# Expert stage of an attention and mixture-of-experts kernel: tiles of 64 slots instead of 128

## What is computed

```python
logits = x @ w_gate                       # 1792 x 768 @ 768 x 8
e_idx = np.argmax(logits, axis=1)
...
for e in range(E):
    mask = e_idx == e
    h = np.maximum(x[mask] @ w1[e], 0.0)  # 768 -> 1024
    ye = h @ w2[e]                        # 1024 -> 768
    out[mask] = gate_w[mask, None] * eom[mask, e, None] * ye
```

## Time and profile before

| | us |
|---|---|
| median of 3 runs (lowest to highest) | 1076.08 (1074.73 to 1076.96) |
| profiled execution, its own time | 1077.28 |
| span of the profiled execution | 1075.2 |
| TensorE busy | 1055.4 |
| VectorE / ScalarE / GpSimd busy | 560.1 / 428.6 / 256.6 |
| expert stage, first matmul to last | 765.9 to 1067.7 |

### The profile page before, as it was taken

One profiled execution on the slowest core, in us unless ns is written; L12 is line 12 of the kernel. 1 busy time (PEld: TensorE's weight loads), 2 busy tenths in 40 slices (PEclk: granted clock), 3 DMA queues, 4 the chain that ended last, 5 costly groups with the idle time before them and its releaser, 6 DMA issues.

```text
span 1075.2 us, 20947 instructions
## 1 busy us (share of the span) xinstructions
PE 1055.4 (98%) x8120; PEld 621.7 (58%) x8121; DVE 560.1 (52%) x830; ACT 428.6 (40%) x611; POOL 256.6 (24%) x219
## 2 busy tenths in 40 slices
PE   7999999999999999999999999999999999899997
PEld 3444334444555555555555555556787887778785
DVE  7899999984433344433333321004455456266651
ACT  6788888886211111111111220001254444246531
POOL 5887878841000000000000100000121121122222
PEclk9999999999999999999999999999999999999999
DMA  6267867541411111111100432000366357357620
GB/s 159 59 140 139 174 146 166 118 95 36 149 44 51 54 51 54 49 54 58 59 30 1 162 104 81 36 29 30 137 221 247 118 209 246 106 199 286 215 95 19
DMA packets 117610, 118.89 MB, mean 111 GB/s; under 512 B 71600, under 2 KB 93486, under 8 KB 117536
## 3 DMA queue, kind: packets, MB, share of 16 engines
q1 hardware_dynamic: 113952, 106.37, 33.9%
q0 software_dynamic: 3168, 11.02, 2.9%
q10 hardware_dynamic: 416, 0.47, 0.2%
HBM read 99.49 MB, written 13.85 MB: 105 GB/s over the span
## 4 chain that ended last, share of the span: by engine, by line
PE 83%; POOL 8%; issue 7%; ACT 1%; DVE 0%; DMA 0%; POOLq 0%; ACTq 0%
PE ps L1695 30%; PE ps L1710 15%; PE ps L1766 14%; PE ps L1774 13%; PE ps L1591 5%; POOL arena L662 3%; PE ps L1565 2%; POOL arena L648 1%; PE ps L1754 1%; POOL arena L652 1%; POOL arena L669 1%; PE ps L1542 1%; PE ps L1582 1%; PE ps L1567 1%; DMA arena<-in_qk 0%
## 5 line engine op out<-in xcount | busy, mean ns | idle before, releaser
L1695 PE MATMUL ps<-arena 128*128 128x448 f16 x1728 | 328.8, 352 | 0.0
L1695 PEld LDWEIGHTS ps<-arena 128*128 128x128 f16 x1728 | 168.2, 98 | 156.1 <-issue 0.5
L1710 PE MATMUL ps<-arena 128*128 128x392 f16 (+1 forms) x996 | 165.3, 329 | 0.0
L1766 PE MATMUL ps<-arena 128*128 128x128 f16 x2592 | 149.1, 220 | 2.9 <-DVE arena L1267 2.9
L1766 PEld LDWEIGHTS ps<-arena 128*128 128x128 f16 x2592 | 147.5, 98 | 5.6 <-DVE arena L1267 3.3
L1774 PE MATMUL ps<-arena 128*128 128x384 f16 x864 | 146.3, 326 | 0.0
L1710 PEld LDWEIGHTS ps<-arena 128*128 (+1 forms) x996 | 97.3, 98 | 66.9
L1267 DVE SCALAR_TENSOR_TENSOR arena<-arena 128x768 f16<-128x768 f32 (+1 forms) x112 | 112.8, 1067 | 38.3 <-ACT arena L973 37.5
L940 ACT ACTIVATE arena<-ps 128x448 f32<-128x448 f32 x48 | 26.1, 543 | 257.8 <-PE ps L1695 257.8
L1591 PE MATMUL ps<-arena 128*128 128x448 f32 x288 | 126.6, 562 | 0.0
L1241 DVE SCALAR_TENSOR_TENSOR arena<-ps,arena 128x448 f32<-128x448 f32 x48 | 30.0, 625 | 171.5 <-PE ps L1695 92.7
(11 more groups left out here) (184 smaller groups left out, 962.7 us busy)
## 6 DMA issues: line engine op xcount, KB each, us to landing
arena<-in_moe_w SPq DMA_DIRECT2D x48, 512.0 KB, 3.8
arena<-in_moe_w SPq DMA_DIRECT2D x64, 384.0 KB, 3.9
arena<-in_qk SPq DMA_DIRECT2D x23, 448.0 KB, 4.5
y_parts<-arena SPq DMA_DIRECT2D x16, 384.0 KB, 2.3
arena<-sums_inv SPq DMA_DIRECT2D x48, 112.0 KB, 2.9
arena<-in_v SPq DMA_DIRECT2D x24, 192.0 KB, 2.9
arena<-in_moe_w_gate SPq DMA_DIRECT2D x12, 384.0 KB, 4.4
arena<-in_moe_w_val SPq DMA_DIRECT2D x12, 384.0 KB, 5.5
```

Source lines behind the costliest of these rows:

```text
L1695: last = nc.tensor.matmul(ps[:, 2 * (b % 2) + g, 0:S], up_w[s][:, g, c, wl], xt[:, b * KC + c, xl], start=(c == 0 and wl + xl == 0), stop= ...
L1710: last = nc.tensor.matmul(ps[:, 4 + 2 * s + h, 0:cols], gt[:, f, gl, bass.ds(t * 128, 128)], wo[:, f, wl, h, 0:cols], start=(f == 0 and gl ...
L1766: last = nc.tensor.matmul(ps[:, b, k * 128:(k + 1) * 128], w1_s[s][:, c, wl, f * 128:(f + 1) * 128], x_t[:, xl, c], start=(c == 0 and k == ...
```

## The change

A tile has 64 slots instead of 128, and an expert has at least three tiles. Of a tile's 128 gathered rows, 64 are the high parts and 64 the low parts of its tokens (`y_dram` is read as half rows of 1536 bytes, and `row_idx` holds twice the row's number plus 0 or 1). Six transposes turn them, and the first layer has 64 moving columns for each matmul. In the second layer the hidden values are 64 columns of weights; the matmul for the left half of the output columns goes to PSUM partitions 0 to 63 and that for the right half to 64 to 127 of the same bank, one after the other as a pair. So one eviction of 384 columns and one scatter of 128 half rows empties a tile, the last one too. The pieces of the next expert's weights are split in its predecessor's first three tiles: 5, 5 and 4 of them (0, 7 and 7 for expert 0), no longer in its own. Room is made for 49 tiles, so routing's tables grow from 22 to 49 entries for each token tile.

```diff
-CONST_COLS = 468
+CONST_COLS = 511
+SLOTS = 64
+SLOT_TILES = 49
...
-        x_rows = ym.take(128, 2 * DM, F16)
-        x_t = ym.take(128, 2 * DM, F16).rearrange("p (l c m) -> p l c m", l=2, c=KC)
+        x_rows = ym.take(128, DM, F16)
+        x_t = ym.take(128, DM, F16).rearrange("p (c l m) -> p c l m", l=2, c=KC)
...
-        hid = m2.take(128, F2, F32)
-        hid_t = m2.take(128, 2 * F2, F16).rearrange("p (b l c m) -> p b l c m", b=2, l=2, c=4)
+        hid = m2.take(128, F2 // 2, F32)
+        hid_t = m2.take(128, F2, F16).rearrange("p (b l c m) -> p b l c m", b=2, l=2, c=4)
...
-        out_rows = Region(xt_at, xt_at + 6144).take(128, DM, F32)
+        out_rows = Region(xt_at, xt_at + 6144).take(128, HALF_DM, F32)
...
-                many = eng.value_load(counts_i[0:1, bass.ds(e, 1)], min_val=1, max_val=TT)
+                many = eng.value_load(counts_i[0:1, bass.ds(e, 1)], min_val=3, max_val=2 * TT)
...
-                tile(e, s, before, True)
-                with eng.If(many > 1):
+                for i in range(3):
+                    tile(e, s, before + i, i)
+                with eng.If(many > 3):
                     if is_at(e, 0):
-                        with eng.Fori(0, many - 1) as i:
-                            tile(e, s, i, False)
+                        with eng.Fori(2, many - 1) as i:
+                            tile(e, s, i, None)
                     else:
-                        with eng.Fori(1, many) as i:
-                            tile(e, s, before + i, False)
+                        with eng.Fori(3, many) as i:
+                            tile(e, s, before + i, None)
...
+        def pieces_ahead(e, i):
+
+            if i is None or is_at(e, E - 1):
+                return ()
+            bounds = (0, 0, 7, PIECES) if is_at(e, 0) else (0, 5, 10, PIECES)
+            return tuple(range(bounds[i], bounds[i + 1]))
...
-                nc.gpsimd.indirect_dma_start(out=x_rows, out_offset=None, in_=y_dram,
+                nc.gpsimd.indirect_dma_start(out=x_rows, out_offset=None, in_=y_halves,
...
-                nc.gpsimd.indirect_dma_start(out=out, out_offset=bass.IndirectOffsetOnAxis(ap=scatter_idx, axis=0),
+                nc.gpsimd.indirect_dma_start(out=out_halves, out_offset=bass.IndirectOffsetOnAxis(ap=scatter_idx, axis=0),
...
-            for h in range(2):
-                cols = slice(h * HALF_DM, (h + 1) * HALF_DM)
-                pool.wait_ge(half_idx_ready, 2)
-                pool.wait_ge(last_out_ready, h + 1)
...
+            scatter(last)
...
             def hidden(g, b):
 
                 act.wait_ge(hid_sum, 2 * g + b + 1)
                 wait(act, hid_lo_ready, 2 * g)
-                nc.scalar.activation(hid[:, b * 512:(b + 1) * 512], ps[:, b, :], ACT.Relu, scale=1.0 / S_OP)\
+                nc.scalar.activation(hid[:, b * 256:(b + 1) * 256], ps[:, b, 0:256], ACT.Relu, scale=1.0 / S_OP)\
                     .then_inc(hid_ready, 1)
...
-                if first:
-                    split_high(e, s, range(KC + 5, PIECES) if is_at(g, 0) else range(KC, KC + 4))
+                if is_at(g, 0):
+                    split_high(e, s, range(KC + 5, PIECES))
                 hidden(g, 0)
-                if first and not is_at(g, 0):
-                    split_high(e, s, range(KC + 4, PIECES))
                 hidden(g, 1)
-                if first and not is_at(e, E - 1):
-                    split_high(e + 1, 1 - s, range(KC))
+                split_high(e + 1, 1 - s, pieces_ahead(e, i))
...
-            stage("past", nc.vector.tensor_tensor(past3, per_tile(pos, 23), per_entry(cst[:, 305:328], 23), ALU.is_ge))
+            stage("past", nc.vector.tensor_tensor(past3, per_tile(pos, SLOT_TILES + 1), per_entry(cst[:, 319:369], SLOT_TILES + 1), ALU.is_ge))
...
-                if is_at(e, 1) and first:
-                    split_low(e, s, range(3, KC))
-                if first:
-                    split_low(e, s, range(KC + 5, PIECES) if is_at(g, 0) else range(KC, KC + 4))
+                if is_at(g, 0):
+                    split_low(e, s, range(KC + 5, PIECES))
                 hidden_split(g, 0)
-                if first and not is_at(g, 0):
-                    split_low(e, s, range(KC + 4, PIECES))
                 hidden_split(g, 1)
+                ahead = pieces_ahead(e, i)
+                split_low(e + 1, 1 - s, ahead[:2])
                 rows_out(g + 1)
-                if first and not is_at(e, E - 1):
-                    split_low(e + 1, 1 - s, range(3 if is_at(g, 0) else KC))
+                split_low(e + 1, 1 - s, ahead[2:])
...
-                last = nc.tensor.matmul(ps[:, 2, 0:110], at_slot[:, t * 128:(t + 1) * 128], quant[:, t * 110:(t + 1) * 110],
+                last = nc.tensor.matmul(ps[:, 2, 0:5 * SLOT_TILES], at_slot[:, t * 128:(t + 1) * 128],
+                                        quant[:, t * 5 * SLOT_TILES:(t + 1) * 5 * SLOT_TILES],
...
-                for l in range(2):
-                    for c in range(KC):
-                        last = nc.tensor.transpose(ps[:, bank + l, :].bitcast(F16)[:, c * 128:(c + 1) * 128],
-                                                   x_rows[:, l * DM + c * 128:l * DM + (c + 1) * 128], ident)
-                    last.then_inc(rows_turned, 1)
+                for c in range(KC):
+                    last = nc.tensor.transpose(ps[:, bank, :].bitcast(F16)[:, c * 128:(c + 1) * 128],
+                                               x_rows[:, c * 128:(c + 1) * 128], ident)
+                last.then_inc(rows_turned, 1)
...
-                            last = nc.tensor.matmul(ps[:, b, k * 128:(k + 1) * 128], w1_s[s][:, c, wl, f * 128:(f + 1) * 128],
-                                                    x_t[:, xl, c], start=(c == 0 and k == 0 and xl + wl == 0),
+                            last = nc.tensor.matmul(ps[:, b, k * SLOTS:(k + 1) * SLOTS], w1_s[s][:, c, wl, f * 128:(f + 1) * 128],
+                                                    x_t[:, c, xl], start=(c == 0 and k == 0 and xl + wl == 0),
...
-            def down_k(s, h, k):
+            def down_k(s, k):
 
                 for hl, wl in PASSES:
-                    last = nc.tensor.matmul(ps[:, 4 + h, 0:HALF_DM], hid_t[:, k // 4, hl, k % 4],
-                                            w2_s[s][k][:, wl, h * HALF_DM:(h + 1) * HALF_DM],
-                                            start=(k == 0 and hl + wl == 0), stop=(k == 7 and hl == 1))
+                    for h, rows in enumerate(HEAD_ROWS):
+                        last = nc.tensor.matmul(ps[rows, 4, 0:HALF_DM], hid_t[:, k // 4, hl, k % 4],
+                                                w2_s[s][k][:, wl, h * HALF_DM:(h + 1) * HALF_DM],
+                                                start=(k == 0 and hl + wl == 0), stop=(k == 7 and hl == 1))
```

More of the change, by code:

```diff
@@ L201, in attention_moe_moe_kernel @@
         mx, key, gw, eom, weight = (te(n=TT) for _ in range(5))
-        shifted, eq, chosen, ez, sig_e, ex, total, incl, base, before = (te() for _ in range(10))
+        masks = te(n=10 * TE)
+        shifted, eq, chosen, ez, sig_e, ex, total, incl, base, before = (masks[:, x * TE:(x + 1) * TE] for x in range(10))
+        past = masks[:, 0:TT * (SLOT_TILES + 1)]
         chosen16 = te(F16)
@@ L224, in attention_moe_moe_kernel @@
         EARLY_SPLIT = 5
-        tok = te(n=22)
-        tok_half = [te(U32, 22) for _ in range(2)]
-        half_idx = [ym.take(128, 1, U32) for _ in range(2)]
+        sent_mark = ym.take(128, 1, U32)
         w2_home = [ym.take(128, 2 * DM, F16) for _ in range(EARLY_SPLIT - 1)] + [fixed.take(128, 2 * DM, F16)]
@@ L593, in _ @@
             for t in (TT - 2, TT - 1):
-                sp.dma_start(y_dram[t * 128:(t + 1) * 128, :], x_rows).then_inc(y_blank, 16)
+                for l in range(2):
+                    sp.dma_start(y_dram[t * 128:(t + 1) * 128, l * DM:(l + 1) * DM], x_rows).then_inc(y_blank, 16)
             def store_y(t, s):
@@ L766, in _, with tile @@
             gather(1)
-            nc.gpsimd.memset(half_idx[0], 4096).then_inc(second_sent, 1)
-            def tile(e, s, before, first):
+            nc.gpsimd.memset(sent_mark, 4096).then_inc(second_sent, 1)
+            def tile(e, s, before, i):
                 if not is_at(before, -1):
@@ L1030, in _ @@
             last = last_tile(act)
[L1031 to L1036 removed]
+            rows_done(last)
         @block.vector
@@ L1382, in _ @@
             need("tiles")
-            stage("tiles", nc.vector.tensor_scalar(tiles_e, tiles_e, 1.0, None, ALU.add))
+            stage("tiles", nc.vector.tensor_scalar(tiles_e, tiles_e, 1.0, 3.0, ALU.add, ALU.max))
             need("sig")
@@ L1386, in _ @@
             need("tiles")
-            stage("ends", nc.vector.tensor_tensor_scan(ends_e, cst[:, 456:464], tiles_e, 0.0, ALU.mult, ALU.add))
+            stage("ends", nc.vector.tensor_tensor_scan(ends_e, cst[:, 498:506], tiles_e, 0.0, ALU.mult, ALU.add))
             need("sig")
@@ L1440, in _ @@
```

(28 more changed lines are left out.)

141 lines of the change are left out of this document (59 added, 82 removed).

## The result

The changed kernel takes 1082.61 us in the median (1080.5 to 1085.29) where the kernel before takes 1076.52 on the same chip (1074.73 to 1077.47): a ratio of 1.0061, 95% interval 1.0042 to 1.0080. It is 0.6% slower. The profiled executions are 1084.57 us (span 1082.8) and 1077.28 us (span 1075.2), so the two traces differ by 7.6 us of span.

A forecast was written before the change was run, and what follows sets the result against it. TensorE, busy 98% of the span, bounds the kernel. Tiles of 283.5 us plus stage waits give 301.2 against 301.7; with routing's +2.8 and 1 us for the clock, +3.3 us: 1080 us, range 1062 to 1094.

The forecast's parts named there:

- One tile: Expert stage on TensorE: a 64-slot tile takes 4.19 + 3.90 + 0.33 + 0.44 = 8.86 us, 32 tiles 283.5 us.
- R1: Rival, second layer: the paired matmuls take turns, 124.8 us more over 32 tiles, 1195 us; chance 8%.
- R2: Rival, faster: shape changes cost nothing when both shapes have all 128 rows, 14.1 us less, 1066 us; chance 9%.
- R3: Rival, faster: first-layer matmuls run at 25.2 ns also at 64 columns, 18 us less, 1062 us; chance 8%.
- (a): Before the stage: larger routing tables make TensorE wait 2.3 us and lengthen the table matmuls by 0.8, +2.8 us in all.
- (b): Stage's first tile: the second gather lands 9.15 us after the first matmul but is wanted after 6.4, +2.8 us.
- (c): Expert 0: VectorE's seven pieces of expert 1 overrun the second tile, so the third tile's hidden rows wait, +1.9 us.
- (d): First tile of each later expert: VectorE's splits and the copy the next tile needs just fit; 0.5 us for all.
- R4: Rival, slower: VectorE and ScalarE don't fit in tiles that split ahead, 0.5 us in each of 20, 1090 us; chance 17%.
- (e): Experts' boundaries: loading two counts is less hidden by queued matmuls, 5 x 0.5 = 2.5 us.
- (f): Expert 4's first tile: the loop over expert pairs jumps back; 3.1 + 1.2, and 1.4 for the clock, 5.7 us.
- (g): Experts 6 and 7 skip the loop body with its 400 TensorE instructions; expert 6's skip costs 4.3 us.

## Why the prediction was right, and where its steps failed

The forecast was 1080 us and slower, at 58%. The median is 1082.6; against the profiled execution the sum gave 1080.6 and the trace has 1084.6. So the sign was right and the sum 4 us short, the net of larger errors. The sign owes something to luck. Of the 7.6 us by which the spans differ, 3.3 and 2.5 come from two things that no term names; the terms that the sum has come to 1.8 us as measured, and such a timing can hardly tell that from no change.

- **One tile** was right to 0.03 us: 8.86 against 8.89. Its terms hold one by one: 29.1 ns for 64 columns on the line through 128 and 384 columns (4.19 us and a change of 0.11 is 4.30, seen 4.31), 162.5 ns for a pair, 0.11 us for a change of shape. R1, R2 and R3 are out. Taking the pair's price from pairs on row halves was sound.
- **(a) routing** was right: 1.97 us of wait where 2.3 stood, table matmuls of 1.68 us where 0.86 + 0.8 stood, and 2.9 in all for 2.8. In these 2.9 are 0.4 us by which TensorE comes later to the table in this trace, ahead of the wait; the terms alone are 2.5.
- **(b)** was mis-sized: 1.5 for 2.8. The gather was still issued when the last rows were stored, but landed 7.9 us after the stage's first matmul and not 9.15: it was issued 4.6 us after it instead of 5.0, and took 3.3 us instead of 4.1. It moves half the bytes; that this is the reason wasn't tested. Most of the 1.5 is something else that was not seen: VectorE's hidden split stands behind three weight pieces in the first tile (0.93 us, in the row of 774.02). VectorE's rows there:

```profile
770.60 2.70 DVE L1255 SCALAR_TENSOR_TENSOR arena<-arena 128x768 f16<-128x768 f32 x3 [0.60 <-ACT arena L971]
773.22 0.28 DVE L1463 CAST arena<-arena 128x256 f16<-128x256 f32 x1
```

- **(c)** was right, 1.6 for 1.9. **(d)** fitted as laid out: the second tiles start without a wait on VectorE's copy, so R4 is out. **(e)** was over-sized: five boundaries cost 0.9 us in all, not 2.5. GpSimd's waits did not carry over to TensorE.
- **(f) and (g)** were right in kind and place, and 11.8 us for 11.0 with the clock. The half clock behind the jump costs more than before: the first layer there takes 7.03 us for 4.37, where the kernel before had 9.64 for 8.20.
- **Missing: stops on code in straight lines**, 3.3 us, and most of the 0.6 of the table's last row. "Runs ahead of its code" was thought of for branches alone. The step that failed is the sum over a tile's terms as if the instructions were always there; the tile's instructions come nearly twice as fast.
- **Missing: the tail**, 2.5 us, of which 2.2 are the closing drain. "The end loses one of two half scatters and gains nothing" counted the transfers at the end, and not that the closing drain counts all of them.

## What to carry to other kernels

When a change makes instructions shorter and more of them, price their number too: the array's changes of shape in a tile, the code's blocks, and what the end pays for each transfer. Put operations of one shape together, if what they wait for has landed by then; a wait made elsewhere can cost the clock behind it as well. Where the page names a releaser that had long ended, look for a packet on the instruction queue, and shift the code to test it. A difference of a few microseconds between two such kernels can be stops of another length at the same places: compare tile by tile before you put it down to the edit.

## What the runs showed of the hardware

- A change between 128*128 and column halves costs TensorE 0.114 us with all 128 rows in use (8.66, 8.89 and 9.12 us for 2, 4 and 6 in a tile).
- Two matmuls of 384 columns on the two column halves take the time of one, 162.5 ns, and TensorE took the partner from four places further on in the program.
- Straight code of 64-column matmuls, two instructions in 29 ns, stopped TensorE at fixed places of the code, for 1.0 and 2.25 us in the changed kernel and up to 2.5 us in the other traces; it went on 1.2 to 1.6 us behind the end of a 16 KB packet of code.
- GpSimd's closing drain takes 0.082 us longer for each indirect transfer that was issued (3.341 us with 40 of them, 5.546 with 67, 5.627 with 68).
- TensorE's clock fell to the 1.2 GHz level in or behind every gap of 2.9 to 4.1 us in the stage, and its work behind the gap took 1.2 to 2.7 us longer for it. At gaps of 1.8 to 2.7 us it went either way: it fell at 1.82 us (26th tile with six changes) and at 2.17 us (eighth tile without the branch), and not at 2.18 us (eighth tile of the changed kernel), nor at 2.63 us (ahead of expert 7 with the halves apart).
